# One core, attention and two MLPs: a fifth of the squares and the attention parts move to GpSimd, VectorE keeps fewer attention steps

## The reference

```
h = mab(I, x);  y = mab(x, h)       # mab(q, kv): softmax(q kv^T / sqrt(C)) kv, sum + 1e-9
h1 = y @ w_in                        # first MLP
g  = (a0 + a1 h1 + a2 h1^2 + a3 h1^3) / (1 + |b0| |h1| + |b1| h1^2 + 1e-6)
z  = g @ w_out
h2 = z @ w2_in                       # second MLP
out = (h2 * cos(h2)) @ w2_out
```

## Time and profile before

| | us |
|---|---|
| median of 3 runs | 2683.2 (2681.61 to 2685.51) |
| profiled execution, its own time | 2681.58 |
| its span | 2679.7 |

### The profile page before, as it was taken

One profiled execution on the slowest core, in us unless ns is written; L12 is line 12 of the kernel. 1 busy time (PEld: TensorE's weight loads), 2 busy tenths in 40 slices (PEclk: granted clock), 3 DMA queues, 4 the chain that ended last, 5 costly groups with the idle time before them and its releaser, 6 DMA issues.

```text
span 2679.7 us, 38024 instructions
## 1 busy us (share of the span) xinstructions
PE 2610.2 (97%) x10691; PEld 1760.5 (66%) x10691; DVE 2390.3 (89%) x2818; ACT 2483.1 (93%) x3175; POOL 1753.8 (65%) x953
## 2 busy tenths in 40 slices
PE   8699999999999999999999899999999999999998
PEld 5355555555555555555555577777777777777776
DVE  4699999999999999999999888888888888888887
ACT  5599999999999999999999799999999999999997
POOL 0166666666666666666666677777777777777776
PEclk9799999999999999999999999999999999999999
DMA  8000000000002000000000000000000000000000
GB/s 221 15 12 7 11 7 11 7 11 7 11 16 69 8 11 7 11 7 11 7 11 4 0 8 12 11 11 13 12 11 11 11 11 11 11 11 11 11 11 15
DMA packets 25686, 45.50 MB, mean 17 GB/s; under 512 B 2888, under 2 KB 11880, under 8 KB 25384
## 3 DMA queue, kind: packets, MB, share of 16 engines
q1 hardware_dynamic: 25640, 44.92, 5.6%
HBM read 16.99 MB, written 12.78 MB: 11 GB/s over the span
## 4 chain that ended last, share of the span: by engine, by line
PE 62%; ACT 24%; issue 8%; DVE 5%; DMA 1%; ACTq 0%; POOL 0%; DVEq 0%; SPq 0%; POOLq 0%
PE bank L1125 21%; PE bank L1113 20%; PE bank L976 9%; ACT work L468 7%; ACT work L485 7%; PE bank L983 7%; ACT work L473 6%; DVE work L741 3%; ACT work L486 2%; PE bank L991 2%; ACT abs_third L486 1%; ACT tokens_t L492 1%; PE bank L1104 1%; PE bank L907 1%; DVE bank L723 1%
## 5 line engine op out<-in xcount | busy, mean ns | idle before, releaser
L399 POOL TENSOR_TENSOR act_lo<-work,act_hi 128x960 fp32r<-128x960 f32 (+1 forms) x416 | 724.4, 1744 | 340.3 <-ACT act_hi L563 329.8
L360 POOL TENSOR_TENSOR work<-work 128x960 f32<-128x960 f32 x278 | 622.8, 2240 | 410.5 <-DVE work L732 410.5
L983 PE MATMUL bank<-work,v 128*128 128x480 f32 x1664 | 749.4, 572 | 5.4 <-ACT tokens_t L492 0.2
L976 PE MATMUL bank<-part_hi,stack_now 96*128 96x480 f32 x2496 | 659.7, 399 | 28.5 <-DVE work L741 12.3
L976 PEld LDWEIGHTS bank<-part_hi,stack_now 96*128 96x128 f32 x2496 | 439.2, 189 | 339.7 <-DVE work L741 275.8
L872 DVE SCALAR_TENSOR_TENSOR work<-work,bank 128x960 f32<-128x960 int32 x416 | 479.7, 1153 | 169.5 <-PE bank L1125 168.9
L723 DVE SCALAR_TENSOR_TENSOR bank<-bank,over_sigma,work 128x960 f32<-128x960 f32 x416 | 508.9, 1223 | 34.5 <-PE bank L976 25.1
L741 DVE SCALAR_TENSOR_TENSOR work<-bank,coef_a,work 128x960 f32<-128x960 f32 x416 | 503.0, 1209 | 1.6
L550 ACT ACTIVATE work<-bank 128x960 int32<-128x960 f32 x416 | 405.0, 974 | 102.7 <-PE bank L1113 102.2
L485 ACT ACTIVATE work<-bank,made 128x960 f32<-128x960 f32 x416 | 454.7, 1093 | 26.1 <-PE bank L976 26.1
L878 DVE TENSOR_TENSOR work<-work,bank 128x960 f32<-128x960 f32 x416 | 477.3, 1147 | 0.0
(11 more groups left out here) (119 smaller groups left out, 2741.9 us busy)
## 6 DMA issues: line engine op xcount, KB each, us to landing
x_group<-tokens_t SPq DMA_DIRECT2D x52, 240.0 KB, 2.2
out_dram<-work SPq DMA_DIRECT2D x52, 240.0 KB, 2.4
x_ring<-in_x_dram SPq DMA_DIRECT2D x40, 240.0 KB, 6.5
work<-in_x_dram SPq DMA_DIRECT2D x12, 240.0 KB, 6.0
stack_now<-stack_next SPq DMA_DIRECT2D x8, 288.0 KB, 3.0
work<-in_moe_w_in_dram SPq DMA_DIRECT2D x1, 1024.0 KB, 15.6
w_raw<-in_moe_w_in_dram SPq DMA_DIRECT2D x1, 1024.0 KB, 5.0
v<-in_moe_w_out_dram SPq DMA_DIRECT2D x2, 0.5 KB, 14.0
```

The costliest lines, as they stand in the source:

```text
L360: nc.gpsimd.tensor_tensor(quot[k % 3], square[k % 3], abs_h[k % 3], ALU.add).then_inc(den_ready, 1)
L399: nc.gpsimd.tensor_tensor(act2_lo[:, k % 2, w], angle[k % 4][:, w], act2_hi[:, k % 2, w].bitcast(F32), ALU.subtract).then_inc(act2_parted, 1)
L976: mm = pe.matmul(place_out[:, t, :], stack_now[:, i, w], part_hi[0:K3, place, :], start=start, stop=stop, skip_group_check=not start)
L983: mm = pe.matmul(sums, v[:, 2 * u + t, :], g[:, t * GROUP:(t + 1) * GROUP], start=(2 * u + t == 0), stop=(2 * u + t == CHUNKS - 1))
```

## The change

The squares of the last 96 of each 480 columns are made by POOL as magnitude times magnitude (`square_rest`); ACT squares 384 of 480 (768 of 960 columns). The scale that ACT put into the square goes into its logarithm, and the scalars for it are derived in another way. DVE's attention steps are max, shift, sum, reciprocal, norm and one copy, each in slot 3 of a step of its own (the 1e-9 is a 33rd column of the sum). The exponentials and the sum lie in SBUF instead of PSUM. The norm writes one copy instead of three; PE makes the three row blocks by twelve ordinary matmuls of 32 output rows instead of four transposes of 96. DVE copies the result from PSUM to `att_t`, and POOL makes the high part and the low part from there, ahead of and behind a denominator.

```diff
-SCORE, MAX, SHIFT, EXP2 = -14, (-13, 0), (-12, 3), -11
-SUM, ADD_EPS, INVERT, NORM, TURN = (-10, 1), (-10, 2), (-10, 3), (-9, 3), -8
-PART_HI, PART_LO = (-8, 3), (-7, 3)
+SCORE, MAX, SHIFT, EXP2 = -14, (-13, 3), (-12, 3), -11
+SUM, INVERT, NORM, TURN = (-11, 3), (-10, 3), (-9, 3), -8
+KEEP_ATT, PART_ATT = (-8, 3), -7
...
+            def square_rest(n0, k):
+                n = n0 + k
+                pool.wait_ge(square_ready, n + 1)
+                pool.wait_ge(abs0_ready, n + 1)
+                pool.wait_ge(abs1_ready, n + 1)
+                rest = halves(abs_h[k % 3])[:, :, OWN:]
+                nc.gpsimd.tensor_tensor(halves(square[k % 3])[:, :, OWN:], rest, rest, ALU.mult).then_inc(square_parted, 1)
...
+                pool.wait_ge(square_parted, n + 1)
                 nc.gpsimd.tensor_tensor(quot[k % 3], square[k % 3], abs_h[k % 3], ALU.add).then_inc(den_ready, 1)
+            def high_att(place):
+                nc.gpsimd.tensor_copy(part_hi[0:K3, place, :], att_t[0:K3, :]).then_inc(att_hi_ready, 1)
+            def low_att(g, place):
+                pool.wait_ge(att_hi_ready, g + 1)
+                low = part_hi[2 * M:K3, place, :]
+                nc.gpsimd.tensor_tensor(low, att_t[2 * M:K3, :], low.bitcast(F32), ALU.subtract).then_inc(att_parted, 1)
+                pool.wait_ge(att_parted, g + 1)
...
+                    if new:
+                        pool.wait_ge(att_kept, n0 // GROUP_UNITS + g + 1)
+                    if there:
+                        square_rest(n0, k + DEN)
+                    if new:
+                        high_att(g % PLACES)
+                    if there:
+                        denominator(n0, k + DEN)
+                    if new:
+                        pool.wait_ge(den_ready, n0 + (k + DEN) + 1)
+                        low_att(n0 // GROUP_UNITS + g, g % PLACES)
...
-                nc.scalar.activation(halves(square[k % 3]), hid, ACT.Square, scale=made[:, 8:9]).then_inc(square_ready, 1)
+                nc.scalar.activation(halves(square[k % 3])[:, :, 0:OWN], hid[:, :, 0:OWN], ACT.Square).then_inc(square_ready, 1)
...
-                nc.vector.tensor_tensor(att[:, :, :, :], thrice, inv, ALU.mult).then_inc(att_ready, 1)
+                nc.vector.tensor_tensor(att[:, :, :], att_exp[:, :, 0:M], over_m(sub_inv[:, :]), ALU.mult).then_inc(att_ready, 1)
...
+            def keep_att(g, place):
                 dve.wait_ge(att_turned, g + 1)
+                if not isinstance(g, int) or g >= 1:
+                    dve.wait_ge(att_parted, g)
+                nc.vector.tensor_copy(att_t[0:K3, :], spare[0:K3, 0:GROUP]).then_inc(att_kept, 1)
...
                 for j in range(GROUP_SUBS):
-                    thrice = att[:, j, :, :].rearrange("p r m -> p (r m)")
-                    mm = pe.transpose(spare[0:K3, j * SUB:(j + 1) * SUB], thrice, ident[0:SUB, 0:SUB])
+                    for r in range(3):
+                        mm = pe.matmul(spare[r * M:(r + 1) * M, j * SUB:(j + 1) * SUB], att[:, j, :], ident[0:SUB, 0:SUB],
+                                       start=True, stop=True)
```

More of the change, by code:

```diff
@@ L131, in bass_set_attention_two_mlps @@
         x_group = sb("x_group", [P, GROUP])
-        att = sb("att", [SUB, GROUP_SUBS, 3, M])
+        att = sb("att", [SUB, GROUP_SUBS, M])
+        att_exp = sb("att_exp", [SUB, GROUP_SUBS, M + 1])
         ident = sb("ident", [P, P])
@@ L140, in bass_set_attention_two_mlps @@
         held_b = sb("held_b", [P, 2])
-        made = sb("made", [P, 9])
-        over_sigma = sb("over_sigma", [P, 2])
+        made = sb("made", [P, 6])
+        over_c2 = sb("over_c2", [P, 2])
         neg_max = sb("neg_max", [P, 2])
@@ L153, in bass_set_attention_two_mlps @@
         sub_inv = sb("sub_inv", [SUB, GROUP_SUBS])
+        own = sb("own", [P, M])
+        ind_t = sb("ind_t", [C, M])
+        peak = sb("peak", [1, M])
+        run_max = sb("run_max", [P, STEPS + B])
+        step_sum = sb("step_sum", [P, STEPS])
         h_sum = at(low_at, "h_sum", [P, B, C])
@@ L160, in bass_set_attention_two_mlps @@
         chosen = at(low_at + 3072, "chosen", [P, B, 3, M])
[L161 to L165, removed]
+        att_t = at(low_at + 4 * UNIT, "att_t", [P, GROUP])
         x_ring = at(next_at, "x_ring", [SUB, RING_NEXT, GROUP_SUBS * C])
@@ L345, in _ @@
                                     pattern=[[-1, P]], channel_multiplier=1).then_inc(ident_ready, 1)
-            def denominator(n0, k):
+            def square_rest(n0, k):
                 n = n0 + k
-                later = not isinstance(n, int)
                 pool.wait_ge(square_ready, n + 1)
@@ L353, in denominator @@
                 pool.wait_ge(abs1_ready, n + 1)
-                if later or n >= 3:
+                rest = halves(abs_h[k % 3])[:, :, OWN:]
+                nc.gpsimd.tensor_tensor(halves(square[k % 3])[:, :, OWN:], rest, rest, ALU.mult).then_inc(square_parted, 1)
+            def denominator(n0, k):
+                n = n0 + k
+                if not isinstance(n, int) or n >= 3:
                     pool.wait_ge(act_ready, n - 2)
@@ L359, in denominator @@
                     pool.wait_ge(folded_in, B * PIECES if n == 2 else PIECES)
+                pool.wait_ge(square_parted, n + 1)
                 nc.gpsimd.tensor_tensor(quot[k % 3], square[k % 3], abs_h[k % 3], ALU.add).then_inc(den_ready, 1)
+            def high_att(place):
[5 more added lines that the diff above has]
+                pool.wait_ge(att_parted, g + 1)
             def units(n0, ks):
                 for k in ks:
-                    if k + DEN >= 0 and exists_unit(n0 + (k + DEN)):
-                        denominator(n0, k + DEN)
+                    g = group_due(k, PART_ATT)
+                    new = g is not None and exists(n0 // GROUP_UNITS + g)
+                    there = k + DEN >= 0 and exists_unit(n0 + (k + DEN))
+                    if new:
[5 more added lines that the diff above has]
+                    if there:
+                        denominator(n0, k + DEN)
+                    if new:
+                        pool.wait_ge(den_ready, n0 + (k + DEN) + 1)
+                        low_att(n0 // GROUP_UNITS + g, g % PLACES)
+            pool.wait_ge(att_kept, 1)
+            high_att(0)
+            low_att(0, 0)
             units(0, range(-DEN, 1))
@@ L462, in s2_exponent @@
                 act_.wait_ge(s2_shifted, g + 1)
-                nc.scalar.activation(spare[0:SUB, GROUP_SUBS * M:2 * GROUP_SUBS * M].rearrange("p (j m) -> p j m", m=M), att[:, :, 0, :], ACT.Exp, scale=SCALE).then_inc(s2_exp, 1)
+                nc.scalar.activation(att_exp[:, :, 0:M], att[:, :, :], ACT.Exp, scale=SCALE).then_inc(s2_exp, 1)
             def log_den(n0, k):
@@ L467, in log_den @@
                 act_.wait_ge(den_ready, n0 + k + 1)
-                nc.scalar.activation(q, q, ACT.Ln, bias=1.0 + EPS_Q).then_inc(log_ready, 1)
+                nc.scalar.activation(q, q, ACT.Ln, bias=1.0 + EPS_Q, scale=made[:, 5:6]).then_inc(log_ready, 1)
             def invert_den(n0, k):
@@ L507, in units @@
                         invert_den(n0, k + NUM)
[L509 to L512, removed]
+            act_.wait_ge(consts_loaded, 48)
             for k in range(STEPS + 2):
@@ L521, in _ @@
                 if k == BATCH_STEPS + 7:
-                    act_.wait_ge(scales_step, 8)
+                    act_.wait_ge(scales_step, 7)
                 fold = 2 * (k - BATCH_STEPS - 7)
@@ L676, in shift_s2 @@
                     dve.wait_ge(att_turned, g)
-                nc.vector.tensor_tensor(att[:, :, 0, :], s2, over_m(sub_max[:, :]), ALU.subtract).then_inc(s2_shifted, 1)
+                nc.vector.tensor_tensor(att[:, :, :], s2, over_m(sub_max[:, :]), ALU.subtract).then_inc(s2_shifted, 1)
             def sum_s2(g, place):
                 dve.wait_ge(s2_exp, g + 1)
[L681 to L685, removed]
+                nc.vector.reduce_sum(sub_inv[:, :], att_exp[:, :, :], AX_X).then_inc(sum_step, 1)
             def invert(g, place):
-                dve.wait_ge(sum_step, g * 3 + 2)
+                dve.wait_ge(sum_step, g * 2 + 1)
                 nc.vector.reciprocal(sub_inv[:, :], sub_inv[:, :]).then_inc(sum_step, 1)
             def norm_s2(g, place):
-                dve.wait_ge(sum_step, g * 3 + 3)
-                thrice = e2.rearrange("p j (o m) -> p j o m", o=1).broadcast_to([SUB, GROUP_SUBS, 3, M])
-                inv = sub_inv[:, :].rearrange("p (j o q) -> p j o q", o=1, q=1).broadcast_to([SUB, GROUP_SUBS, 3, M])
-                nc.vector.tensor_tensor(att[:, :, :, :], thrice, inv, ALU.mult).then_inc(att_ready, 1)
-            def part_att_hi(g, place):
-                dve.wait_ge(att_turned, g + 1)
[L700 to L706, removed]
+                dve.wait_ge(sum_step, g * 2 + 2)
+                nc.vector.tensor_tensor(att[:, :, :], att_exp[:, :, 0:M], over_m(sub_inv[:, :]), ALU.mult).then_inc(att_ready, 1)
+            def keep_att(g, place):
+                dve.wait_ge(att_turned, g + 1)
```

(12 more changed lines are left out.)

40 lines of the change are left out of this document (19 added, 21 removed).

## The result

| | before | after |
|---|---|---|
| median, us | 2683.65 | 2723.01 (2721.41 to 2724.13, 4 runs) |
| ratio, 95% interval | | 1.0146 (1.0129 to 1.0164) |
| profiled execution / span, us | 2681.58 / 2679.7 | 2723.14 / 2721.3 |
| a group of the first MLP, L998 to L998, L1017 to L1017, mean of 50 intervals | 26.64 | 27.51 |

The change makes the kernel 1.5% slower: 39 us, where +14 was forecast. The sign was right, the size a third. The granted clock is 1.00 in the first MLP as before, and the loss lies there: 0.87 us over 50 intervals between turns is 43.5. Another 1.4 come ahead of the first of them, 3.2 are won behind the last turn, and that makes the 41.6 between the spans.

What follows compares the result with a forecast made beforehand. Bound: the PE-DVE loop of slope, product and quotient, 3.14 us a step. Terms +0.66 - 0.24 - 0.20 - 0.04 + 0.12 gave +0.30 a group, +15 us over 51 intervals: 2697, own range 2686 to 2712, wide range 2676 to 2730.

Steps and rivals of the forecast that it cites:

- The loop of 3.14 without ACT: First MLP, plain steps: slope, product and quotient on PE and DVE set 3.14 us; lighter ACT leaves it unchanged.
- The sum moved out of slot 1: DVE's sum leaves the loop between product and quotient: that step goes from 3.34 to 3.14, -0.20 a group.
- The turn: PE's twelve matmuls take 1.0 us where four transposes took 0.34: +0.66 a group, all on the path.
- -0.04 for the copy: DVE's high-part copy moves behind the new turn, beside slope's 0.75, leaving that step at 3.21 for 3.25.
- Rivals 1 and 5: 1: turn takes 0.80, POOL never late, no change, 2682, chance 0.22. 5: turn runs serially, 2763, chance 0.05.
- The wait for y, -0.24: In the turning step L983 waits for ACT's copy of y; fewer ACT squares remove PE's 0.24 a group.
- POOL, "it is 0.25 late, PE's air takes half: +0.12": POOL's denominator behind the low part makes ACT's logarithm 0.25 late; PE's 0.14 of air leaves +0.12 a group.
- The deadline: ACT's logarithm of unit 5 must start by 9.75 after the turn's start, for hidden(8) due at 11.11 + 0.94.
- The lock: DVE's norm, both inputs in SBUF, waits 0.7 for POOL's denominator, hidden by 1.07 us spare in the turning step.
- rival 4: Norm waits a whole POOL denominator on the path: 1.2 a group, up to +60 us, chance 0.06.
- Rivals 2 and 3: 2: ACT was the pacer, faster, 2646, chance 0.12. 3: POOL becomes the bound, 2728 at strip 0.80, chance 0.10.
- my own case: Whole kernel slower by 4 to 28 us, range 2686 to 2712, chance 0.45.

Runs made afterwards that it cites:

- The run of the turn alone: Kernel before, with only PE's four transposes replaced by twelve matmuls of 32 rows: 2716.01 us, ratio 1.0122.
- the run with both edits: Changed kernel with POOL's square and denominator ahead of its wait for DVE's copy, and four transposes of a three-copy norm again: 2670.61 us, ratio 0.9955.
- the best version: Changed kernel with POOL's wait for DVE's copy behind ready work, four transposes, and the low part behind the second denominator: 2662.49 us, ratio 0.9921.

## Why the prediction was wrong in size

- *The loop of 3.14 without ACT:* right. Plain steps are 3.14 in every run, with ACT lighter (ratio 0.9936) or not. The sum moved out of slot 1: 3.34 became 3.14, -0.20 as said.
- *The turn:* right. 0.95 against a forecast of 1.0, so +0.61. Its 24 records start in eight threes about 0.10 apart (604.34, then 604.47, 604.57 and so on to 605.08), as I had counted them. Two terms that I had otherwise come with it: it starts 0.09 later behind the output, and the step behind it is 3.14 for 3.26, -0.12 where I had -0.04 for the copy. The run of the turn alone shows both with the old copy in place, and with four transposes the step is 3.24 again. Together +0.58, against my +0.62. Rivals 1 and 5 fall.
- *The wait for y, -0.24:* failed. It fell only by 0.03 (slope to output 1.68, then 1.65). I costed it as if ACT's relief came alone. ACT's rate was nearly as forecast, 3.03 a step for 3.01, though by another sum: the square gives 0.25, not 0.18, and the moved scale takes 0.10 of it back. What was wrong is where ACT starts from: GpSimd throws it back once a group, and 0.11 a step doesn't make that up before the copy of y. With the relief alone (768 columns in the kernel before) the wait goes, and with the same 3.03 and GpSimd's order changed it goes too (1.41 in both). Without the scale, at 0.2 a step, ACT also makes it.
- *POOL, "it is 0.25 late, PE's air takes half: +0.12":* this step of the prediction failed, and with the y it is the missing 26 us: 0.40 and 0.21 a group above the forecast, 30 us in 50 groups, less the 4 that the turn and the two ends make up. Mechanism, place and culprit were as told, and POOL itself was even quicker (second denominator done 9.63 after the turn, not 10.0; the strip 0.51, not 0.60; busy 856 of 1000 us in the stage, where my 97% also counts the handovers). The deadline was wrong. I followed ACT's own half of the magnitudes to the hidden unit and got 9.75 for the logarithm. DVE's half also waits for the square, takes 0.65 and has maximum and product behind it in the queue: product due at 11.74 less 0.57, 0.20, 0.79 (square's end) and 0.99 (logarithm) is 9.2. The logarithm came at 9.67, and the step lengthened by 0.52 in the mean. ACT's half ended at 616.27, DVE's at 616.50, so even the wait that I followed ended with DVE.
- *The lock:* norm ran 0.28 each time and waited nowhere (rival 4 falls), but it also met nothing: in every group POOL's denominator ended at most 0.05 after norm's start, and the 0.7 of overlap that I had worked out did not come about. Where norm is three times as long, in the run with both edits, it meets POOL's strip, which lasts 0.66 instead of 0.51:

```profile
636.02 0.66 POOL L362 TENSOR_TENSOR work<-abs_third 128x192 f32<-128x192 f32 x1 [0.24 <-DVE abs_third L756]
```

  Norm ran from 635.77 to 636.32. And at the end of the first MLP of the kernel after, the operation of the earlier trace rows comes between two of POOL:

```profile
1539.51 0.53 POOL L359 TENSOR_TENSOR work<-work 128x192 f32<-128x192 f32 x1 [0.54 <-DVE work L755]
1539.71 0.88 DVE L857 TENSOR_TENSOR w_lo<-w_raw,w_hi 128x512 fp32r<-128x512 f32 x1
1540.18 2.49 POOL L371 TENSOR_TENSOR work<-work 128x960 f32<-128x960 f32 x1
```

  It ends 0.55 after the strip (1540.04), as it ended 0.55 after the denominator before, and takes 0.88 for 2.65; the denominator behind it takes 2.49 for 2.24. The rule cited ahead (Trainium skill, SBUF — State Buffer, on the engine ports) fits these rows, GpSimd being the loser in two of them; no run was made for it. That shorter stand of DVE is probably what wins the 3.2 us behind the last turn (PE stood there for 2.89 before, for 1.04 after), but that is read from the rows and no run tests it.
- *Rivals 2 and 3:* plain steps are 3.14 with ACT at 3.03 a step and less, so ACT was not the pacer. Rival 3, POOL as the bound, names the nearest time (2728), but its condition failed, 0.51 and not 0.80 for the strip, and the same work of POOL in another order takes 26.68 a group. That 2723 lies within my wide range of 2676 to 2730 is luck: the range was that wide for rivals that did not come about, and my own case ended at 2712.

The sum as measured, a group: turn +0.61, its later start +0.09, step behind the turn -0.12, late step +0.52, wait for y -0.03, sum -0.20: +0.87, and 0.87 was seen. Two runs undo the terms one at a time: order -0.83 (the late step, and the wait for y with it), turn -0.57; together they give 1.00, not 1.40. How the remaining 0.2 of y in the best version, and the 0.08 behind it, could go was not tried further.

## What to carry to other kernels

A helper engine with idle time is not free: ask what stands behind each of its waits, and put a wait for a late input behind the work that is ready, not ahead of it. When a producer gets later, take the deadline through every consumer's queue, the one with the most in-order work behind it decides; and check that relief counted elsewhere (here ACT's) is not spent making up for the delay. Where one engine's own work bounds a step, as PE's does in the turn, what is added there is paid almost in full (0.57 of 0.61).

## What was not expected of the hardware

- Twelve fp32 matmuls of 32 rows in three row blocks, 24 records, took 0.95 us in each of the five kernels that have them; four blocks and 16 records took 0.57.
- A scale read from memory costs ACT 0.09 to 0.10 us an instruction, independent of the function (square 0.94 to 0.85, logarithm 0.90 to 0.99).
- PE picks up a waiting hidden unit 0.25 after DVE's end (616.50 to 616.75), not the 0.05 of the slope; and an output that waited delays the next weights by 0.08.
- A GpSimd instruction that meets a DVE operation with two inputs in SBUF ends 0.15 less than its own length after it: the strip of 0.51 after 0.36, the denominator of 2.24 after 2.08.
